# Another order at the attention's chunk edges, and a first tile of the second expert layer made before the counts

## The reference

```python
def _moe_ref(x, w_skip, w_gate, w1, w2):      # first layer
    do_compute = x @ w_skip > 0               # the other rows are passed on as they are
    e_idx = argmax(x @ w_gate)
    y = gate * (relu(x @ w1[e]) @ w2[e])      # e, gate: of the row's chosen expert
    out[do_compute] = x + y
...
def _moe2_ref(x, modality_id, w_gate, modality_bias, w1, w2):   # second layer
    e_idx = argmax(x @ w_gate + modality_bias[modality_id])
    out = gate * (relu(x @ w1[e]) @ w2[e])
```

## Time and profile before

| what | value |
|---|---|
| median of 3 runs | 1529.11 us (1528.56 to 1531.15) |
| profiled execution, its own time | 1530.26 us |
| its span | 1528.5 us, mean granted TensorE clock 0.991 |
| TensorE busy | 1484.9 us, 97% of the span |
| DVE / ACT / POOL busy | 1010.1 / 770.9 / 396.0 us |
| attention | 0 to about 730 us |
| first expert layer | about 741 to 1034 us |
| second expert layer | 1048.7 to 1510 us, then the last rows are stored |

### The profile page before, as it was taken

How to read it: one execution, slowest core, us unless ns; L and a number is a source line. 1 busy time by engine, 2 the same in 40 slices (tenths; PEclk the granted TensorE clock), 3 DMA queues, 4 the chain that set the end, 5 groups by cost and what they waited for, 6 DMA issues and landing times.

```text
span 1528.5 us, 34462 instructions
## 1 busy us (share of the span) xinstructions
PE 1484.9 (97%) x11777; PEld 1290.2 (84%) x11777; DVE 1010.1 (66%) x2375; ACT 770.9 (50%) x1504; POOL 396.0 (26%) x370
## 2 busy tenths in 40 slices
PE   8999999999999999999899999998999999999995
PEld 7778878788878888788799999997888888888884
DVE  7989977899779988977666666673333333333332
ACT  6676766676667767665344444442332333333331
POOL 4133322334223424212222222221511211211211
PEclk9999999999999999999999999999999999999998
DMA  5311030212212020200533353322211111111110
GB/s 118 97 32 62 28 98 28 64 40 56 84 32 64 28 84 27 85 30 31 168 107 134 134 179 129 103 94 69 97 49 49 42 64 48 42 46 53 42 46 24
DMA packets 57743, 107.27 MB, mean 70 GB/s; under 512 B 17863, under 2 KB 32210, under 8 KB 57612
## 3 DMA queue, kind: packets, MB, share of 16 engines
q0 software_dynamic: 18192, 58.13, 11.0%
q1 hardware_dynamic: 39420, 47.48, 10.8%
HBM read 75.63 MB, written 31.49 MB: 70 GB/s over the span
## 4 chain that ended last, share of the span: by engine, by line
PE 83%; DVE 5%; issue 4%; DMA 3%; ACT 2%; POOL 1%; SPq 0%; POOLq 0%; DVEq 0%; ACTq 0%
PE pO L1359 25%; PE pS L1625 11%; PE pO L1637 10%; PE pS L1563 9%; PE pO L1546 9%; PE pS L1348 7%; PE pO L1639 5%; PE pM L1625 4%; DVE AH L1031 3%; DMA raw<-in_v_dram 2%; PE pT L1600 1%; DMA token_rows<-xrow,dest 1%; PE pT L1407 1%; DVE AL L1033 1%; PE pT L1495 1%
## 5 line engine op out<-in xcount | busy, mean ns | idle before, releaser
L1033 DVE TENSOR_TENSOR AL<-A,AH 128x512 fp32r<-128x512 f32 (+1 forms) x400 | 307.1, 768 | 13.7
L1359 PE MATMUL pO<-AH,VH 64*128 64x512 f32 (+1 forms) x1520 | 298.9, 384 | 8.0 <-DVE xT L941 6.1
L1359 PE MATMUL pO<-AH,VL 64*128 64x512 f32 (+1 forms) x1520 | 297.5, 382 | 0.0
L1359 PE MATMUL pO<-AL,VH 64*128 64x512 f32 (+1 forms) x1520 | 297.3, 382 | 0.0
L672 ACT ACTIVATE R<-pS 128x512 f32<-128x512 f32 (+1 forms) x400 | 213.3, 587 | 157.3 <-PE pS L1348 140.1
L1031 DVE CAST AH<-A 128x512 fp32r<-128x512 f32 (+1 forms) x400 | 233.8, 584 | 43.1 <-ACT A L681 42.3
L681 ACT ACTIVATE A<-R 128x512 f32<-128x512 f32 (+1 forms) x400 | 229.2, 624 | 17.7 <-DVE AL L1033 17.5
L1637 PE MATMUL pO<-VL,AH 128*128 128x512 f32 x640 | 232.4, 399 | 0.0
L1298 DVE SCALAR_TENSOR_TENSOR AL<-pS,AH 128x512 fp32r<-128x512 f32 x120 | 82.9, 692 | 186.0 <-ACT AH L862 185.3
L1639 PE MATMUL pO<-VL,AL 128*128 128x256 f32 x640 | 179.4, 280 | 0.0
L1359 PEld LDWEIGHTS pO<-AH,VH 64*128 64x128 f32 x1520 | 147.2, 184 | 35.3 <-issue 10.8
(11 more groups left out here) (218 smaller groups left out, 2416.1 us busy)
## 6 DMA issues: line engine op xcount, KB each, us to landing
raw<-in_w_dram POOLq DMA_DIRECT2D x22, 1024.0 KB
A<-token_rows SPq DMA_DIRECT2D x21, 536.0 KB, 3.6
uT<-in_u_dram SPq DMA_DIRECT2D x16, 512.0 KB
A<-in_w2t_dram POOLq DMA_DIRECT2D x8, 1024.0 KB
xin<-token_rows SPq DMA_DIRECT2D x24, 268.0 KB
raw<-in_v_dram SPq DMA_DIRECT2D x4, 1152.0 KB, 5.8
raw<-in_v_dram SPq DMA_DIRECT2D x4, 768.0 KB, 7.9
raw<-in_z_dram SPq DMA_DIRECT2D x8, 368.0 KB
```

The source lines that it names most:

```text
L1033: v_.tensor_tensor(AL[k % NBUF][:, 0:n], A[k % NA][:, 0:n], AH[k % NBUF][:, 0:n].bitcast(F32), ALU.subtract).then_inc(al_ready, 1)
L1359: last = t_.matmul(pO[:, (KD * r + d) * QW:(KD * r + d) * QW + n], vv[rows, vo + k * D + d * P:vo + k * D + (d + 1) * P], a[k % NBUF][rows ...
```

## The change

At the attention's edges: POOL scatters the last chunk before it multiplies with u. DVE places rows behind slot 0 (was 2) and adds the sums ahead of key tile 3 (was behind it). ACT copies the second half of `xrow` in slot 0 (was 1) and casts V's second half in slots 5 to 9 (was 1, 3, 5, 7, 9). TensorE makes the second transposes and the prefix counts in slot 6 (was 7). V's second half is loaded in two pieces, the first of them (four key tiles) as soon as two units of the first half are split.

Between the layers: the second layer's first tile (the lead) takes up to 512 rows that the attention alone gave to the expert that comes first. Their number and the row where they end are worked out at the start of the first layer (`plan_second`), and POOL writes 512 pad rows behind them before any first-layer tile is scattered. SP loads the lead tile without waiting for the counts, but no second tile before them. TensorE transposes the lead into two banks of `pO`, runs its groups with a ring of `pS[0]`, `pS[1]` and pT, and makes the last first-layer tile's prefix counts between its groups 1 and 2. DVE does that tile's routing and `finish_groups(1)` between its halves. The loops then begin at tile 1, and the lead's rows are subtracted from the first expert's count. In later turns ACT casts the next weights behind half 4, not behind half 7.

```diff
+                sp.wait_ge(vl_ready, 2)
+                load_v(0, VHALF, VHALF + 4)
                 sp.wait_ge(vl_ready, VU // 2)
-                load_v(0, VHALF, KT)
+                load_v(0, VHALF + 4, KT)
...
+                            sp.wait_ge(vl_ready, VU * b + VU + 2)
+                            load_v(b + 1, VHALF, VHALF + 4)
                             sp.wait_ge(vl_ready, VU * b + VU + VU // 2)
-                            load_v(b + 1, VHALF, KT)
+                            load_v(b + 1, VHALF + 4, KT)
...
                     sp.wait_ge(early_ready, ph + 1)
-                    sp.wait_ge(rows_stored, 64 * CHUNKS)
-                    full = sp.value_load(early[0:1, ph:ph + 1], min_val=0, max_val=2)
-                    e = expert(ph * E)
-                    if ph == 1:
+                    if ph == 0:
+                        sp.wait_ge(rows_stored, 64 * CHUNKS)
+                        full = sp.value_load(early[0:1, ph:ph + 1], min_val=0, max_val=2)
+                        with sp.If(full > 0):
+                            with sp.Fori(0, full) as t:
+                                load_x(t, t * rows_in)
+                    else:
+                        e = expert(E)
                         sp.wait_ge(gcols_made, E)
-                        sp.sem_inc(sp_passed, 1)
-                    with sp.If(full > 0):
-                        with sp.Fori(0, full) as t:
-                            load_x(t, within(e * CAP + t * rows_in, 0, GR * CAP - rows_in))
+                        sp.wait_ge(lead_padded, 16)
+                        load_x(0, within(e * CAP, 0, GR * CAP - rows_in))
...
+                if g > 1:
+                    scatter_chunk(g - 1)
                 if g > 0:
                     times_u(g)
-                if g > 1:
-                    scatter_chunk(g - 1)
...
+                if ph == 1:
+                    next_weights(E, 0, True)
+                    scatter_out(0)
...
-                pool.wait_ge(early_ready, 2)
+                if ph == 0:
+                    pool.wait_ge(early_ready, 2)
+                    row = pool.value_load(lead[0:1, 1:2], min_val=0, max_val=GR * CAP - TT2)
+                    pool.dma_start(xs[ds(row, TT2), :].rearrange("(p s) d -> p s d", p=P),
+                                   pad_row[:, None, :].to_broadcast([P, SUB2, ROW])).then_inc(lead_padded, 16)
+                    wait(lead_padded, 16)
...
-                        elif c == QC - 2:
-                            v_high(b + 1, VU // 2 + p // 2)
                         elif c == QC - 1:
                             z_high(b + 1, p // 2)
+                    if p >= VU // 2 and b < B - 1 and c == QC - 2:
+                        v_high(b + 1, p)
...
-                    if p == 1 and g > 1:
+                    if p == 0 and g > 1:
...
+                with act.If(total0 > 0):
+                    act.wait_ge(first.shifted, total0)
+                    s_.activation(ex[:, 0:SUB, 1, :], lsh[:, 0:SUB, 1, :], ACT.Exp).then_inc(first.exp, 1)
+                    act.wait_ge(first.y_out, total0 + 1)
+                    act.wait_ge(first.stored, STORED - 32 + 32 * total0)
+                    s_.copy(x2s, x2a).then_inc(first.staged, 1)
+                for f in range(NF):
+                    h_high(0, f, hring_lead)
+                    if 3 <= f < 3 + WP:
+                        split_high(E + 1, 1, f - 3)
+                take_half(1, 1, 0, pT[:, :])
+                take_half(1, 1, 1, pT[:, :])
+                keep_marks(1, 1)
+                for s in range(SUB2):
+                    low_part(0, 0, s)
...
+                    if k == 2 * AHEAD - 3 and g > 0:
+                        add_sums(g)
...
-                        if p == AHEAD - 2:
-                            add_sums(g)
                         if p == 7:
                             pick_experts(g)
                         if p == 8:
                             row_meta(g)
                             set_gates(g)
-                        if p == 2 and g > 1:
+                        if p == 0 and g > 1:
...
+                rows_by, base_by = cnt[:, es], base[:, es]
+                if ph == 1:
+                    by_turn(tiles_t[:, :], rows_by)
+                    f(v_.tensor_tensor(tiles_t[:, 0:1], tiles_t[:, 0:1], lead_f[:, :], ALU.subtract))
+                    by_turn(base_t[:, :], base_by)
+                    rows_by, base_by = tiles_t[:, :], base_t[:, :]
...
+                f(v_.tensor_tensor(cnt[:, E:GR], base[:, E:GR], group0[:, E:GR], ALU.subtract))
                 plan_counts()
                 plan_turns()
                 plan_order()
-                plan_first(1)
+                by_turn(base_t[:, :], cnt[:, E:GR])
+                f(v_.tensor_scalar(lead_f[:, :], base_t[:, 0:1], float(TT2), None, ALU.min))
+                by_turn(tiles_t[:, :], base[:, E:GR])
+                v_.tensor_copy(lead[:, 0:1], lead_f[:, :])
+                v_.tensor_copy(lead[:, 1:2], tiles_t[:, 0:1]).then_inc(early_ready, 1)
...
+                low_half(0, 0, 0, pO[:, 0:QW])
+                low_half(0, 0, 1, pO[:, QW:2 * QW])
+                total0 = dve.value_load(cum[0:1, 0, E:E + 1], min_val=0, max_val=64)
+                with dve.If(total0 > 0):
+                    pick_expert(total0)
+                h_low(0, 0, hring_lead)
+                with dve.If(total0 > 0):
+                    place_tile(total0)
+                h_low(0, 1, hring_lead)
+                h_low(0, 2, hring_lead)
+                finish_groups(1)
+                for f in range(3, NF):
+                    h_low(0, f, hring_lead)
+                low_half(1, 1, 0, pT[:, :])
+                low_half(1, 1, 1, pT[:, :])
+                add_parts(0, 0)
+                lo = 1
...
-                        if p == 7:
+                        if p == 6:
...
+                transpose_half(0, 0, pO[:, 0:QW])
+                transpose_half(0, 1, pO[:, QW:2 * QW])
+                keep_warm(pO[:, 2 * QW:3 * QW], 24)
+                pe.wait_ge(wl_ready, WP * (E + 1))
+                pe.wait_ge(q.xt_split, 2)
+                layer1(0, 0, 0, 0, hring_lead)
+                layer1(0, 0, 0, 1, hring_lead)
+                total0 = pe.value_load(cum[0:1, 0, E:E + 1], min_val=0, max_val=64)
+                with pe.If(total0 > 0):
+                    prefix_x2(total0)
+                layer1(0, 0, 0, 2, hring_lead)
+                for f in range(3, NF):
+                    layer2(0, 0, f - 3)
+                    layer1(0, 0, 0, f, hring_lead)
+                pe.wait_ge(q.h_split, NF + 6)
+                transpose_half(1, 0, pT)
+                layer2(0, 0, 5)
+                layer2(0, 0, 6)
+                transpose_half(1, 1, pT)
+                layer2(0, 0, 7)
                 pe.wait_ge(cum_ready, 2)
-                lo = 0
+                lo = 1
```

More of the change, by code:

```diff
@@ L112, in bass_attention_two_moe @@
         load_from = sb("load_from", [P, 2, E], I32)
+        lead_f = sb("lead_f", [P, 1])
+        lead = sb("lead", [P, 2], I32)
         ZH = sb("ZH", [P, ZW], F32R)
@@ L412, in _ @@
                         with sp.If(lo < hi):
-                            first = sp.value_load(load_from[0:1, ph, at:at + 1], min_val=0, max_val=64)
+                            first = lo if ph else sp.value_load(load_from[0:1, ph, at:at + 1], min_val=0, max_val=64)
                             e = expert(at + ph * E)
+                            row = e * CAP
+                            if ph and at == 0:
+                                row = row + sp.value_load(lead[0:1, 0:1], min_val=0, max_val=TT2)
                             sp.wait_ge(padded, 16 * (at + 1 + ph * E))
@@ L565, in _, with scatter_out @@
             scatter_chunk(CHUNKS)
+            def scatter_out(t):
+                for s_ in range(SUB2):
+                    wait(PH[1].y2_out, SUB2 * t + s_ + 1)
+                    g_.indirect_dma_start(out, bass.IndirectOffsetOnAxis(tok_at2[:, s_:s_ + 1], 0), xrow[:, s_, 0:D], None,
+                                          bounds_check=N - 1, oob_is_err=False).then_inc(PH[1].stored, 16)
             for ph in range(2):
                 q = PH[ph]
+                if ph == 1:
+                    next_weights(E, 0, True)
+                    scatter_out(0)
                 pool.wait_ge(cum_ready, ph + 1)
@@ L595, in _ @@
                                                               bounds_check=GR * CAP - 1, oob_is_err=False).then_inc(q.stored, 16)
[L596 to L597 removed]
+                            if turn_ != E:
+                                with pool.If(t == lo):
+                                    ahead()
                             if ph == 1:
[L599 to L604 removed]
+                                scatter_out(t)
+                    if turn_ != E:
+                        with pool.Else():
+                            ahead()
                 if ph == 0:
@@ L1601, in transpose_half, with layer1 @@
```

(28 more changed lines are left out.)

244 lines of the change are left out of this document (102 added, 142 removed).

## The result

The changed kernel takes 1523.38 us as a median of 7 runs (1521.33 to 1525.46), the kernel before 1529.20 (7 runs, 1528.32 to 1531.15). The ratio is 0.9962 [0.9952, 0.9973]: 5.8 us faster, where 13.8 were forecast, and outside the range of 1511 to 1521. The profiled execution took 1522.68 us.

A forecast was written before the change was run, and what follows sets the result against it. TensorE, busy nearly always, was taken as the bound, with gains only in its holes: 5.0 us in the attention plus 8.8 between the layers, 13.8 from 1530.26, gives 1516.5, as a median 1515.3 us; range 1511 to 1521.

The forecast's parts named there:

- Scatter before the product with u: Attention edges: scatter starts some 6 us earlier, saving TensorE 0.7 us; the product queued behind it costs nothing.
- rival B: Attention: two subtractions more in DVE's crowded slots 7 to 9 cost 8 us over three batches; 1523.3 us, chance 0.05.
- The stores of the last chunk: Attention edges: ACT's wait for these stores goes with the earlier scatter, and TensorE's 0.74 us behind it; 0.7 us gained.
- V's second half: Attention: casts in slots 5 to 9 gain 2.4 us over three chunks; the earlier first-batch load gains 0.6 us.
- The sums one key tile earlier: Attention edges: 1.1 us gained in chunk 1; later, placing's 0.93 replaces 1.07 us, giving 0.4 us together.
- Prefix counts at slot 6: Attention: TensorE waits 1.8 us for the one-hot at chunk 16 without losing time; zero overall, up to 2 us lost.
- Rival D: Attention: prefix at slot 6 makes all 19 chunks wait for the one-hot; at 1 us each 1534 us, chance 0.02.
- Between the layers: Second expert layer's start: layer 1 begins at 1038.3, not 1048.68; 10.4 us less three costs, 8.8 us gained (5 to 10.5).
- The second tile: Second layer: its rows land 0.2 us after TensorE wants them; 0.7 us lost was taken (0 to 3).
- C: Second layer: second tile's rows come 3 us late, pad and load each 1.5 us longer; 1518.3 us, chance 0.08.
- E: Between the layers: the lead does nothing, its first rows or casts arriving as late as the counts did; 1524.1 us, chance 0.03.
- The clock: Low clock at the first layer's start may shift 2 us either way; full clock between layers; clock or unnamed: chance 0.02.

The follow-up runs named there:

- thin_product: Changed kernel, order unchanged, but POOL's product with u covers 32 of each 512 columns; 1519.26 us (later stages are other work), attention ends at 722.36.
- product_first: Changed kernel with POOL's product with u ahead of the scatter again, all else as changed; 1508.94 us, 0.9873 of the kernel before.
- pf_mix: Changed kernel with the product ahead of the scatter again, and second transposes and prefix counts in slot 7 for chunk 16 alone; 1508.89 us, 0.9873.
- lead_only: Kernel before with the lead tile alone, every attention edge as before; 1518.33 us, 0.9933 of the kernel before.
- edges_only: Kernel before with the attention edges' new order alone, no lead tile; 1534.10 us, 1.0031 of the kernel before.

## Why the prediction was wrong

**Scatter before the product with u: the failed step.** The prediction asked what is queued behind the scatter and whether the product would come too late for TensorE's routing: "Six us to spare, so nothing". That was right, `thin_product` shows it, and it was the wrong question. The move also changes what POOL does at the moment when DVE makes AL. At ten of eighteen edges it turned two halves that began 1.6 to 2.3 us apart into one block. At all eighteen it put that block where DVE already has a cast or an AL under way, which then stood still for the whole block, and in c = 2 and c = 4 for the V or Z units right behind it too. That costs the attention 14.2 us (738.06 against 723.87).

A row for it was at hand, the cast of 4.41 us beside three subtractions. The product of 2.73 us at chunk 5 looked harmless and was, in its old place. The Trainium skill (SBUF — State Buffer, section "SBUF: two separate sides") says that a DVE operation with two SBUF inputs and a GpSimd operation that reads SBUF exclude each other for a whole instruction, and that the one that starts first goes first. AL has two SBUF inputs. The trace agrees that the two exclude each other: AL ends 0.49 to 0.57 us behind POOL's last operation nine times of nine. It differs in the rest: by the timeline AL or the cast began first, by 0.2 to 0.7 us, and was the one held, for a row of two to four operations and not for one. The prediction weighed this sharing for the V casts alone (rival B), took the number of POOL's operations, which stayed, and never laid POOL's new order beside DVE's. So B came near the time by chance (1523.3 against 1523.38): its place, slots 7 to 9, was not where the time went.

**The stores of the last chunk, 0.7 us: mis-sized.** The placing of rows behind slot 0 and the early scatter were counted by TensorE's visible wait. In `product_first`, placing is worth 7.0 us by the ratio when the sums stay early, 2.0 (3.8 less 1.8) when they are late too. A part of this is a need that the change itself creates, ACT's copy in slot 0; how large a part was not run.

**V's second half, 2.4 us in three chunks and 0.6 in the first batch.** In `product_first` chunks 3, 8 and 13 are 4.3 us shorter than before. The experiment gives 2.0 by the ratio and 5.9 at the attention's end, the first batch's load included: of the right order, and its size is left open. In the changed kernel the wait at 32.15 fell from 1.21 to 0.50, as taken.

**The sums one key tile earlier.** Chunk 1: 1.1 us predicted, 1.07 seen (the wait of 1.26 is 0.19). In the later chunks 0.4 were predicted; chunks 5, 10 and 15, behind the short ones, are 4.5 us shorter in `product_first`. Not all is the sums, but the argument that 1.07 us is exchanged for 0.93 was too strict: what placing takes at slot 0 is not missing at the edge.

**Prefix counts at slot 6.** The forecast saw the one wait that comes, at chunk 16 (1.13 us at 603.04 in `product_first`; 1.8 was the forecast), and that it costs nothing: `pf_mix` takes it away and gains nothing. It missed the other side: slot 6 is what makes the transposes ready for ACT's copy in slot 0, worth 2.3 us. Rival D, slower by this slot, did not occur, though the edges alone ended on its side of the line, by the product.

**Between the layers, 8.8 us: right, a little low.** `lead_only` gives 10.2 by the ratio. In the traces, the stretch from the end of the attention to the last matmul went from 774.65 us (735.16 to 1509.81) to 764.93 (738.06 to 1502.99), 9.7 less. Layer 1 starts 6.3 us after the load's issue at 1034.11, taken as 6.2. The second tile cost 0.59 + 0.26 us (1059.45, 1064.98), taken as 0.7; planning took 2.85 us (1046.24 to 1049.09) inside the tile, hidden. Twenty tiles stayed. Rivals C and E did not occur. The costs taken for the pad writes (3 and about 4 us) stand in no row of before; in the changed kernel the second tile's load follows its pad by 4.75 us, of which nothing shows on TensorE but the pause of 0.59 us ahead of its transposes.

**The clock.** Windows of the changed kernel (us, busy of PE, PEld, DVE, ACT, POOL, granted clock, DMA, GB/s):

```profile
744.00:746.00 2.00, 1.59 (x22) 1.14 (x26) 1.72 (x10) 0.27 (x2) 1.47 (x2) 0.50 0.86 341
...
1034.00:1040.00 6.00, 5.77 (x61) 5.55 (x60) 2.89 (x9) 1.17 (x3) 1.94 (x2) 1.00 0.42 137
```

The low stretch at the first layer's start is still there (0.50, as in the earlier trace rows), and the gap between the layers keeps the upper level. Neither moved the sum.

The account by the ratios: 10.2 us gained by the lead tile (`lead_only`), 9.2 by the other edge edits (`lead_only` to `product_first`; 5.0 were forecast), and 13.6 lost by one block of POOL: 5.8.

## What to carry to other kernels

When an instruction block is moved on POOL, ask not only who waits for it and who queues behind it, but which two-input DVE operations now run beside it, and lay the two engines' timelines over each other at the new place. A stop of this kind shows as a longer instruction, not as a wait: compare the mean and the longest duration of the same line before and after. A block that runs while DVE waits anyway is free, and the same block 2 us later may cost the path most of its length. Ask also what releases the block: here it was harmless while DVE's own result released it, and harmful once it started on its own behind other work of POOL.

## What the runs showed of the hardware

The stop is as long as POOL's row of operations, not one of them: an AL of 0.69 us takes 3.40 beside a product of two halves, 4.69 with one subtraction directly behind and 6.02 with two. A cast with a single input is stopped in the same way (3.19 and 5.59). With 0.75 us between POOL's operations only one holds it up (1.67 us).

For the product the start times tell the two cases apart without an exception: a cast or an AL that began ahead of the block was held for all of it (54 of 54 blocks), and one that began inside the first half was held for one half at a time (57 of 57). Beside rows with V or Z units this is not a rule: nine casts that began 0.1 to 0.6 us inside such a row were held to its end, one of them in the kernel before (3.88 us at 98.39). What makes POOL leave or not leave the gap is open.

DVE's sums, which read one operand from PSUM, are not stopped: all 40 in `product_first` take 0.68 to 0.69 us, 19 of them beside a POOL operation. Indirect DMAs that POOL issues do not stop AL: beside four of them in `product_first`, from 87.39 us on, AL takes 0.69 to 0.74 us.

A wait of TensorE of nearly 2 us in the attention was followed by some 3 us at the lower clock in one execution (1.88 and 1.93 us, `edges_only`) and not in another (1.85 us, the changed kernel).
